# Clamping attention scores into SBUF in one VectorE pass, and issuing the tiles in twos

## What is computed

```
mask = q_bucket[:, :, :, None] == k_bucket[:, :, None, :]
scores = scale * np.matmul(q, k.transpose(0, 1, 3, 2))
scores = np.where(mask, scores, -1000000000.0)
scores = scores - np.max(scores, axis=-1, keepdims=True)
attn = np.exp(scores)
attn = attn / (np.sum(attn, axis=-1, keepdims=True) + 1e-09)
return np.matmul(attn, v).astype(np.float32)
```

## Time and profile before

| | |
|---|---|
| three runs | 782.21, 782.77, 783.22 us; median 782.77 |
| the profiled execution | 782.55 us; span from first to last instruction 780.8 us |
| TensorE matmuls | 759.1 us busy, 97% of the span |
| TensorE weight loads | 583.4 us, 75% |
| VectorE | 486.0 us, 62% |
| ScalarE | 439.5 us, 56% |
| GpSimd | 215.3 us, 28% |

### The profile page before, as it was taken

How to read it: one execution, slowest core, us unless ns; L and a number is a source line. 1 busy time by engine, 2 the same in 40 slices (tenths; PEclk the granted TensorE clock), 3 DMA queues, 4 the chain that set the end, 5 groups by cost and what they waited for, 6 DMA issues and landing times.

```text
span 780.8 us, 11273 instructions
## 1 busy us (share of the span) xinstructions
PE 759.1 (97%) x3712; PEld 583.4 (75%) x3712; DVE 486.0 (62%) x794; ACT 439.5 (56%) x783; POOL 215.3 (28%) x366
## 2 busy tenths in 40 slices
PE   4799999999999999999999999999999999999998
PEld 2666666666666788888888888888888888888886
DVE  4777777777765788889888988861222312232223
ACT  2676677777766788877666888861221212222121
POOL 1655566666663254300000154450000000000000
PEclk9999999999999999999999999999999999999999
DMA  6544455443320123200000133320000100010001
GB/s 148 143 114 106 92 133 129 98 125 93 77 60 1 55 87 102 82 0 0 0 0 0 28 92 97 108 81 0 1 1 0 54 0 0 0 55 0 1 1 54
DMA packets 35084, 43.31 MB, mean 55 GB/s; under 512 B 4192, under 2 KB 23392, under 8 KB 35040
## 3 DMA queue, kind: packets, MB, share of 16 engines
q1 hardware_dynamic: 34752, 42.32, 20.5%
q10 hardware_dynamic: 288, 0.43, 0.2%
HBM read 26.61 MB, written 3.15 MB: 38 GB/s over the span
## 4 chain that ended last, share of the span: by engine, by line
PE 89%; issue 2%; DVE 2%; ACT 2%; DMA 1%; POOL 1%; SPq 1%; ACTq 0%; POOLq 0%; DVEq 0%
PE y_ps L920 33%; PE h_ps L866 11%; PE h_ps L867 11%; PE h_ps L868 11%; PE o_ps L846 8%; PE t_ps L829 7%; PE s_ps L819 4%; PE s_ps L820 3%; ACT probs L448 2%; DVE neg_max L618 1%; DMA probs<-in_k 1%; PE p_ps L803 1%; DVE q_cross L613 1%; PE p_ps L846 1%; POOL exp_bias L397 0%
## 5 line engine op out<-in xcount | busy, mean ns | idle before, releaser
L866 PE MATMUL h_ps<-x_hi,slot 128*128 (+1 forms) x384 | 149.8, 390 | 0.0
L867 PE MATMUL h_ps<-x_lo,slot 128*128 (+1 forms) x384 | 149.5, 389 | 0.0
L712 DVE SCALAR_TENSOR_TENSOR t_abs<-t_abs,h_ps 128x512 f32<-128x512 f32 x48 | 33.0, 689 | 187.1 <-ACT t_abs L520 187.1
L868 PE MATMUL h_ps<-x_hi,slot 128*128 (+1 forms) x384 | 149.5, 389 | 0.0
L520 ACT ACTIVATE t_abs<-h_ps,three_col 128x512 f32<-128x512 f32 x48 | 33.1, 689 | 191.5 <-PE h_ps L868 191.5
L410 POOL TENSOR_TENSOR slot<-w_raw,slot 128x512 fp32r<-128x512 f32 x64 | 81.6, 1293 | 207.0 <-ACT slot L475 206.9
L920 PE MATMUL y_ps<-g_hi,slot 128*128 128x512 f32 x384 | 126.2, 390 | 0.0
L920 PE MATMUL y_ps<-slot,g_hi 128*128 128x512 f32 x384 | 118.2, 389 | 0.0
L448 ACT ACTIVATE probs<-s_ps,exp_bias,exp_scale 128x768 f32<-128x768 f32 x96 | 95.0, 990 | 32.9 <-POOL exp_bias L397 31.5
L618 DVE TENSOR_REDUCE neg_max<-s_ps 128x1 f32<-128x768 f32 x96 | 91.6, 954 | 18.1 <-PE s_ps L820 15.0
L829 PEld LDWEIGHTS t_ps<-ident,probs 128*128 128x128 f32 x576 | 63.5, 143 | 46.4 <-issue 26.2
(11 more groups left out here) (71 smaller groups left out, 1138.4 us busy)
## 6 DMA issues: line engine op xcount, KB each, us to landing
w_raw<-in_moe_w_in SPq DMA_DIRECT2D x32, 256.0 KB, 2.7
w_raw<-in_moe_w_out SPq DMA_DIRECT2D x32, 256.0 KB, 2.8
raw<-in_q SPq DMA_DIRECT2D x16, 192.0 KB, 3.2
v_nat<-in_v SPq DMA_DIRECT2D x16, 192.0 KB, 3.2
raw<-in_k SPq DMA_DIRECT2D x15, 192.0 KB, 3.5
k_main<-q_main SPq DMA_DIRECT2D x15, 192.0 KB, 2.6
k_cross<-q_main SPq DMA_DIRECT2D x15, 192.0 KB, 3.2
k_cross<-q_cross SPq DMA_DIRECT2D x15, 192.0 KB, 2.6
```

What stands on the lines that cost most here:

```text
L866: mm(h_ps[b][:, :], w_hi, x_hi[:, kt, cols], start=(kt == 0), stop=False)
L867: mm(h_ps[b][:, :], w_hi, x_lo[:, kt, cols], start=False, stop=False)
L868: last = mm(h_ps[b][:, :], w_lo, x_hi[:, kt, cols], start=False, stop=(kt == KT - 1))
```

## The change

Scores are made with the opposite sign: the q part is scaled by -1/8 when it is split (a column `scale_col` holds -1/8 for the 64 partitions of q and 1 for those of k), and the mask rows have the sign that makes pairs of different buckets large and positive. On VectorE a clamp takes the place of the maximum: one tensor_scalar from PSUM into `probs`, min with 1e9, its least per row into `least`. The exp then reads `probs` in SBUF with scale -1 and bias `least`. GpSimd's two operations are gone, and scores wait for `clamped` in place of `exped`. `probs` is now written by the clamp, so that the wait for the turn of the tile four before stands ahead of the clamp.

All engines' orders go in steps of two tiles: TensorE scores n, scores n+1, project (j = 0), turn n-3, weigh (two key tiles), turn n-2. Lags, the places of split_hi and split_lo, upper_x and lower_x and the weight halves move with it.

```diff
-    TURN_LAG = 3
-    WEIGH_AT = {1: (0,), 2: (1,), 3: (2, 3), 4: (4,), 5: (5,)}
-    PROJECT_AT = 0
+    WEIGH_AT = {0: (0, 1), 2: (2, 3), 4: (4, 5)}
+    SPLIT_AT = 2
-    LAST_WEIGH = {1: (0, (0,)), 2: (0, (1, 2)), 3: (0, (3,)), 4: (0, (4, 5)),
-                  6: (1, (0,)), 7: (1, (1, 2)), 8: (1, (3,)), 9: (1, (4, 5))}
-    LAST_X = {5: 2 * PAIRS - 4, 10: 2 * PAIRS - 3}
+    LAST_WEIGH = {0: (0, (0, 1)), 2: (0, (2, 3)), 4: (0, (4, 5)), 6: (1, (0, 1, 2)), 8: (1, (3, 4, 5))}
+    LAST_X = 10
-    EARLY_AT = (7, 10)
+    EARLY_AT = (4, 6)
...
-            def bias(n, j):
...
             for i in range(PAIRS):
-                for j in range(2 * TILES):
+                for j in range(0, 2 * TILES, 2):
                     n = 2 * TILES * i + j
-                    bias(n, j)
                     if n >= 1:
                         normalise(n - 1, j - 1)
+                    normalise(n, j)
...
-                nc.scalar.activation(q_main[h % SETS][:, :], raw[i % 2][u][:, :], ACT.Copy).then_inc(hi_made, 1)
+                nc.scalar.activation(q_main[h % SETS][:, :], raw[i % 2][u][:, :], ACT.Identity,
+                                     scale=scale_col[:, 0:1]).then_inc(hi_made, 1)
 
             def exponentials(n, j):
                 r = j % 4
-                act.wait_ge(biased, n + 1)
-                after(act, turned, 2 * (n - 3))
...
+                act.wait_ge(clamped, n + 1)
+                nc.scalar.activation(probs[r][:, :], probs[r][:, :], ACT.Exp, scale=-1.0, bias=least[:, r:r + 1],
                                       accum_out=row_sum[:, r:r + 1]).then_inc(exped, 1)
...
-            def step(i, j):
+            def two_tiles(i, j):
...
+                if t == 0 and h >= 3:
                     upper_x(h - 3)
+                if i == PAIRS - 1 and j == LAST_X:
+                    upper_x(h - 2)
+                if n >= 4:
+                    take_turned(n - 4)
+                if t == SPLIT_AT and h + 2 < NHEAD:
                     split_hi(h + 2)
+                if n >= 3:
+                    take_turned(n - 3)
+                exponentials(n, j)
+                exponentials(n + 1, j + 1)
                 if early_half(i, j):
                     f, half = early_half(i, j)
                     split_weights(0, f, (half,))
...
+                nc.vector.scalar_tensor_tensor(q_cross[c][:, :], raw[h // 2 % 2][h % 2][:, :], scale_col[:, 0:1],
+                                               q_main[c][:, :].bitcast(F32), ALU.mult, ALU.subtract)\
+                    .then_inc(lo_made, 1)
+
+            def clamp(n, j):
+
+                r = j % 4
                 dve.wait_ge(scored, n + 1)
-                nc.vector.tensor_reduce(neg_max[:, j % 4:j % 4 + 1], s_ps[j % 2][:, 0:SEQ], AX.X, ALU.max,
-                                        negate=True)\
-                    .then_inc(maxed, 1)
+                after(dve, turned, 2 * (n - 3))
+                nc.vector.tensor_scalar(probs[r][:, :], s_ps[j % 2][:, 0:SEQ], MASKED, None, ALU.min, ALU.min,
+                                        accum_out=least[:, r:r + 1]).then_inc(clamped, 1)
...
+                if n >= 1:
                     invert(n - 1, j - 1)
+                clamp(n, j)
+                if t == 0 and h >= 3:
                     lower_x(h - 3)
+                if i == PAIRS - 1 and j == LAST_X:
+                    lower_x(h - 2)
+                clamp(n + 1, j + 1)
+                if n >= 3:
+                    take_turned(n - 3)
+                invert(n, j)
+                if j == 0 and i + 1 < PAIRS:
                     threshold(i + 1)
+                if t == SPLIT_AT and h + 2 < NHEAD:
                     split_lo(h + 2)
+                if n >= 2:
+                    take_turned(n - 2)
...
-                after(pe, exped, n - 1)
+                after(pe, clamped, n - 1)
...
                 scores(h, i, u, n, j, t)
+                scores(h, i, u, n + 1, j + 1, t + 1)
+                if j == 0 and i + 1 < PAIRS:
+                    project(i + 1, 0)
+                    project(i + 1, 1)
+                if n >= 3:
+                    turn_probs(n - 3)
                 if i == PAIRS - 1 and j in LAST_WEIGH:
                     weigh(i - 1, *LAST_WEIGH[j])
+                elif 1 <= i < PAIRS - 1:
                     weigh(i - 1, u, WEIGH_AT[t])
...
+                if n >= 2:
+                    turn_probs(n - 2)
```

More of the change, by code:

```diff
@@ L167, in bucket_attention_and_two_mlps @@
         sel_made = sem("sel_made")
+        scale_made = sem("scale_made")
         proj_made = sem("proj_made")
@@ L379, in _ @@
             below(0, 3 * BITS, TINY)
-            below(1, QUAD, 1.0)
+            below(1, QUAD, -1.0)
             nc.gpsimd.memset(ident[:, :], 0.0).then_inc(sel_made, 1)
@@ L441, in split_hi @@
                 after(act, scored, TILES * (h - SETS + 1))
-                nc.scalar.activation(q_main[h % SETS][:, :], raw[i % 2][u][:, :], ACT.Copy).then_inc(hi_made, 1)
+                nc.scalar.activation(q_main[h % SETS][:, :], raw[i % 2][u][:, :], ACT.Identity,
+                                     scale=scale_col[:, 0:1]).then_inc(hi_made, 1)
             def exponentials(n, j):
                 r = j % 4
-                act.wait_ge(biased, n + 1)
-                after(act, turned, 2 * (n - 3))
-                nc.scalar.activation(probs[j % 4][:, :], s_ps[j % 2][:, 0:SEQ], ACT.Exp,
-                                     scale=exp_scale[:, r:r + 1], bias=exp_bias[:, r:r + 1],
+                act.wait_ge(clamped, n + 1)
+                nc.scalar.activation(probs[r][:, :], probs[r][:, :], ACT.Exp, scale=-1.0, bias=least[:, r:r + 1],
                                      accum_out=row_sum[:, r:r + 1]).then_inc(exped, 1)
@@ L503, in _ @@
             for i in range(PAIRS):
-                for j in range(2 * TILES):
-                    step(i, j)
+                for j in range(0, 2 * TILES, 2):
+                    two_tiles(i, j)
             act.wait_ge(poly_in, 32)
@@ L822, in scores, with turn_probs @@
                 last.then_inc(scored, 1)
-            def turn_probs(n, half):
+            def turn_probs(n):
                 pe.wait_ge(normed, n + 1)
-                after(pe, (pt_act_made, pt_dve_made)[half], n)
-                for s in range(GROUP):
-                    c = P * (GROUP * half + s)
-                    last = nc.tensor.transpose(t_ps[half][:, P * s:P * (s + 1)], probs[n % 4][:, c:c + P], ident[:, :])
-                last.then_inc(turned, 1)
+                for half in range(2):
+                    after(pe, (pt_act_made, pt_dve_made)[half], n)
+                    for s in range(GROUP):
+                        c = P * (GROUP * half + s)
+                        last = nc.tensor.transpose(t_ps[half][:, P * s:P * (s + 1)], probs[n % 4][:, c:c + P],
+                                                   ident[:, :])
+                    last.then_inc(turned, 1)
             def weigh(i, g, some):
@@ L874, in step @@
                 scores(h, i, u, n, j, t)
+                scores(h, i, u, n + 1, j + 1, t + 1)
[4 more added lines that the diff above has]
+                    turn_probs(n - 3)
                 if i == PAIRS - 1 and j in LAST_WEIGH:
                     weigh(i - 1, *LAST_WEIGH[j])
-                if 1 <= i < PAIRS - 1 and t in WEIGH_AT:
+                elif 1 <= i < PAIRS - 1:
                     weigh(i - 1, u, WEIGH_AT[t])
-                if j == PROJECT_AT and i + 1 < PAIRS:
-                    project(i + 1, 0)
-                    project(i + 1, 1)
-                if n >= TURN_LAG:
-                    for half in range(2):
-                        turn_probs(n - TURN_LAG, half)
+                if n >= 2:
+                    turn_probs(n - 2)
             project(0, 0)
@@ L889, in _ @@
             for i in range(PAIRS):
-                for j in range(2 * TILES):
-                    step(i, j)
+                for j in range(0, 2 * TILES, 2):
+                    two_tiles(i, j)
             pe.wait_ge(x_ready, 2 * PAIRS - 2)
-            for half in range(2):
-                turn_probs(NTILE - 3, half)
+            turn_probs(NTILE - 3)
             hidden(0, 0, 0, 0)
-            for half in range(2):
-                turn_probs(NTILE - 2, half)
+            turn_probs(NTILE - 2)
             weigh(PAIRS - 1, 0, tuple(range(TILES)))
-            for half in range(2):
-                turn_probs(NTILE - 1, half)
+            turn_probs(NTILE - 1)
             hidden(1, 0, 0, 1)
```

60 lines of the change are left out of this document (17 added, 43 removed).

## The result

The changed kernel takes **769.53 us** (median of 4 runs, 769.2 to 773.71) against 782.49 us for the kernel before on the same chip; the ratio is 0.9847, 95% interval 0.9829 to 0.9864. The profiled execution took 769.31 us with a span of 767.6; the earlier trace rows are of an execution of 782.55 with a span of 780.8. Three executions in the record took 1.7 to 3.4 times the usual time (1520.92 us for lower_x_first, 1363.43 and 2638.63 us for the kernel before) and are left out of all medians here.

A forecast was written before the change was run, and what follows sets the result against it. The prediction took TensorE as the bound, with small holes from waits, and VectorE narrowly setting the new attention step. Its terms, summed to -7.9 us, took the profiled 782.55 us to 774.6, range 768.4 to 782.3.

The forecast's parts named there:

- the ring: VectorE's chain per two-tile step: turn(n-3), second clamp, copy, waiting transposes, next scores; 4.39 us, setting the step.
- rival A: The forecast itself: VectorE's chain sets a two-tile step at 4.39 us; 774.6 us, own range 771 to 779, chance 0.60.
- TensorE's row: TensorE's own work in a two-tile step: two scores bursts, turn, values, turn; 4.22 us, just under VectorE's chain.
- Six pairs: Attention from tile 12 to 84: each pair of heads 27.49 us against 28.88, -8.4 us in all.
- Weight halves: MLP weight splitting on ScalarE behind the exps delays a turn by 0.2 us in four steps, +0.8 in all.
- Ahead of tile 6: Start-up before tile 6's scores: no difference, within 1 us either way; threshold waits for the same DMA.
- First pair: Tile 6 to tile 12: three steps take 13.17 us against 12.91 before, +0.3.
- Last pair: Tile 84 to tile 94: 23.8 us in all against 24.96 before, -1.2.
- Tail: Tile 94's scores to the first hidden matmul: 5.7 us against 5.07, three turns following through VectorE's copies, +0.6.
- B: TensorE's bursts close up to 0.68 us and the clamp needs no second instruction; 768.4 us, chance 0.16.
- C: The clamp in each step is slower than the reduce, 1285 ns instead of 0.94 us; 791 us, chance 0.12.
- D: Waits only move: one more hand-over of 0.14 to 0.2 us per step, step 4.55; 782.3 us, chance 0.12.

The follow-up runs named there:

- lower_x_first: Changed kernel with lower_x (VectorE, low part of x) moved ahead of the first clamp of its step; 769.63 us, ratio 0.9819.
- ring_reduce: Changed kernel plus an unused 384-column VectorE reduce between the second clamp and the copy out of t_ps; 791.9 us, ratio 1.0139.
- ring_column: Changed kernel plus an unused one-column VectorE reduce between the second clamp and the copy out of t_ps; 772.49 us, ratio 0.9899.
- ring_open: Changed kernel with VectorE's half of turned tile n-3 taken out ahead of the second clamp, not behind it; 770.42 us, ratio 0.9835.
- ops_single: The changed kernel's new operations in the order of the kernel before, one tile per step; 773.91 us, ratio 0.9891.
- warm_start: Changed kernel plus ten unread transposes on TensorE behind each of the first two projections; 770.27 us, ratio 0.9844.
- before_warm: Kernel before plus ten unread transposes on TensorE behind each of the first two projections; 783.00 us against 782.65, ratio 1.0004.
- twos_only: The kernel before's operations (reduce, GpSimd's scale and bias, exp from PSUM) in the new two-tile order; 783.03 us, ratio 1.0009.
- combined_warm: Changed kernel with lower_x first, later second threshold, earlier take-out in the first pair, earlier first hidden block, and ten unread transposes behind each of two projections; 763.96 us.

## Why the prediction was right, point by point

The forecast was 774.6 with a range of 768.4 to 782.3; the kernel took 769.53, faster, inside the range and 5 us under the forecast. It was right that TensorE bounds the kernel, that its waits go with the old hand-overs, and that attention's gain passes to the end. It was wrong on what sets the new step: the ring of rival A (4.39) is 4.24, TensorE's row (4.22) is 4.33, and the two errors have opposite signs. That the step came out at nearly the forecast size is in part luck.

- **What bounds it.** Right. TensorE sets the time, the MLPs kept their length, and attention's gain passed to the end one to one.
- **The ring.** Right in its order, 0.15 too long: 4.24 and not 4.39. The clamp to the copy was 0.89 and not 0.94, since the reading of the minimum costs nothing to the next start; from the copy's end to the transposes it was 0.06 (30.55 + 0.55 to 31.16), not 0.14. That row was of a ScalarE copy, and I used it for VectorE. The Trainium skill (VectorE: DVE Perf Modes, "Two Vector instructions with no wait between them") is right that the clamp is two instructions; the price that I put beside it (0.20, from ScalarE) is not VectorE's, whose row is 0.08, under the next start.
- **TensorE's row.** 0.11 too short: 4.33 and not 4.22. The term that failed is the turn in front of values, priced at the 0.63 of a turn in front of scores; it is 0.75. Scores behind scores took 0.72 (0.74 taken). So the step is set by TensorE, not by VectorE "by a little": the same size of step (4.33 against 4.39), with the other engine in front. The steps of ring_reduce, ring_column and ring_open show it.
- **Six pairs.** 27.13 instead of 27.49: the step 0.06 x 6 less, the projection 0.93 instead of 0.85, lower_x 0.22 instead of 0.30. Worth 2.1 us.
- **Weight halves.** The 0.8 us were not there. The mechanism is real: ring_open shows it, at 0.3 a pair. In the changed kernel it delays the turn by 0.07, where I took 0.2, and that lies under the wait for `x_lo`, which I had counted beside it.
- **Ahead of tile 6.** "No difference, within 1 us" failed: -1.59. I read that threshold waits for the same DMA, and it does, but not what is released behind it. Tile 4's start in six kernels puts this on the operations.
- **First pair.** 12.72 instead of 13.17, by the ring's 0.15 three times. **Last pair** -1.56 instead of -1.2. **Tail** +0.63, the forecast size, but by another last wait: I had the last turn wait for VectorE's copy, and it waited for GpSimd's normalise (0.60).
- **Rivals.** A had the right size of step with the wrong engine in front. B's number, 768.4, was nearer than the forecast, but not its reason: bursts don't close up to 0.68 (0.72), and only its free second instruction was so. C fell (clamp 956 ns, 1100 needed). D fell: no further hand-over in the steps with values. What D feared does exist in the first pair, which takes 12.72 where ops_single takes 10.42.

The terms that failed (six pairs, weight halves, ahead of tile 6, first pair, last pair) are -2.1, -0.8, -1.6, -0.5 and -0.4, some 5.3 before rounding, and carry -7.9 to -13.2. Two of the prediction's differences are rounded up: six pairs come to 8.34 and not 8.4, the last pair to 1.14 and not 1.2; its terms as written give -7.8 in place of -7.9.

## What to carry to other kernels

Price a burst by what follows it: here the same six transposes took 0.63 before scores and 0.75 before values, scores 0.72, 0.79 or 0.89, which decided which engine was the bound. Judge an order together with the operations that it orders: twos brought nothing with the old operations and 4.5 us with the new ones, mainly because small GpSimd operations shared a row with weight halves, and TensorE waited for exp behind them. Before making slow first matmuls faster, look for the next stop behind them.

## What the runs showed of the hardware

- On VectorE the reading of the accumulator (80 ns) starts with the next operation and delays it by nothing that shows: 0.88 to 0.89 us from a clamp's start to the next start, 0.87 behind a reduce. ScalarE's lasts 190 ns, and the next operation starts 0.09 us behind its start (103.74 to 103.83).
- A pass that reads 768 PSUM columns, writes 768 to SBUF and keeps their minimum takes 956 ns, the reduce alone took 940 to 960.
- Exp from SBUF with one pointer operand took 932 ns; from PSUM with two it took 990. The Trainium skill (ScalarE: Activation LUTs, "What ACT_TABLE_LOAD costs") gives about 93 ns for each pointer operand; the runs show 58 for pointer and source together and don't part them.
- At the start of the span the granted clock reads 1.00 while 512-column matmuls come every 0.42 us, half the later rate. After a stop of 3.5 to 3.6 us in warm_start and before_warm and of 3.4 us in twos_only it reads 0.50 to 0.53, the lower of TensorE's two levels (1.2 GHz), for some us. After shorter stops it went either way: it fell behind 2.05 us in ring_open, 2.07 in lower_x_first, 1.66 in ring_column and 1.33 in combined_warm, and stayed at 1.00 behind 2.01 in the changed kernel and 1.52 in ring_reduce. So the length of the stop alone doesn't settle it. That part stays open.
